# Gated linear attention fused with two expert layers on one core: the states' part of y goes through PSUM columns of its own, ScalarE copies it out and VectorE adds it to the scores' part

## The reference, cut to what matters

```python
f = 1.0 / (1.0 + np.exp(-f_logit))                    # 4 batches, 8 heads, 768 steps, 48 wide
for t in range(S):
    state = f[:, :, t, :, None] * state + np.einsum('bhd,bhe->bhde', k[:, :, t], v[:, :, t])
    y[:, :, t] = np.einsum('bhd,bhde->bhe', q[:, :, t], state)
x = y.transpose(0, 2, 1, 3).reshape(B * S, H * D)     # 3072 tokens, 384 wide
x = (sigmoid(x @ w_gate) * (x @ w_val)) @ w_out       # hidden width 1536
h = x @ w_in                                          # hidden width 2048
out = (h * sigmoid(1.702 * h)) @ w_out2
```

## Time and profile before

| | us |
|---|---|
| median of 3 runs | 974.91 |
| lowest and highest run | 974.26, 975.66 |
| the profiled execution, its time | 974.81 |
| the profiled execution, its span | 973.1 |
| PE busy in that span | 950.0 (98%) |
| DVE, ACT, POOL busy | 491.0, 303.3, 106.0 |
| mean granted PE clock, as a share of 2.4 GHz | 0.991 |

### The profile page before, as it was taken

The page is one execution under the profiler, slowest core; times in us unless marked ns, Lnnn a source line. Parts: engine busy times, 40 slices in busy tenths (PEclk is TensorE's granted clock), DMA queues, the critical chain, the costliest instruction groups (busy, mean ns, idle before and its releaser), DMA issues.

```text
span 973.1 us, 17708 instructions
## 1 busy us (share of the span) xinstructions
PE 950.0 (98%) x7149; PEld 789.3 (81%) x7149; DVE 491.0 (50%) x876; ACT 303.3 (31%) x621; POOL 106.0 (11%) x125
## 2 busy tenths in 40 slices
PE   7899999999999999999999999999999999999997
PEld 4798988888888887888788888888888888888886
DVE  7787876556554755565332234344343443443433
ACT  3353332222222222222223343333333333332222
POOL 3211211111110111011003440000000000000000
PEclk8899999999999999999999999999999999999999
DMA  5651322211211211121022330020010100100000
GB/s 148 187 174 46 97 69 62 62 42 34 82 43 50 76 52 42 42 75 30 10 90 77 106 105 17 1 66 1 1 65 0 35 31 1 65 1 1 32 1 35
DMA packets 44005, 52.33 MB, mean 54 GB/s; under 512 B 8464, under 2 KB 33808, under 8 KB 43920
## 3 DMA queue, kind: packets, MB, share of 16 engines
q1 hardware_dynamic: 41168, 43.29, 15.3%
q10 hardware_dynamic: 2752, 7.87, 2.7%
HBM read 36.96 MB, written 9.44 MB: 48 GB/s over the span
## 4 chain that ended last, share of the span: by engine, by line
PE 90%; DVE 4%; issue 2%; SPq 1%; ACT 1%; DMA 0%; DVEq 0%
PE up_ps L966 16%; PE up_ps L968 16%; PE up_ps L967 16%; PE out_ps L966 12%; PE out_ps L968 11%; PE out_ps L967 11%; PE att_ps L959 3%; PE att_ps L926 2%; PE att_ps L948 1%; PE turn_ps L905 1%; PE att_ps L938 1%; DVE w_lo L766 1%; ACT act_hi L630 1%; DVE prod L712 1%; DVE act_f L814 0%
## 5 line engine op out<-in xcount | busy, mean ns | idle before, releaser
L966 PE MATMUL up_ps<-x_hi,w_hi 128*128 128x512 f32 (+1 forms) x792 | 294.5, 372 | 5.2 <-DVE x_lo L759 2.7
L968 PE MATMUL up_ps<-x_hi,w_lo 128*128 128x512 f32 (+1 forms) x792 | 293.0, 370 | 0.0
L967 PE MATMUL up_ps<-x_lo,w_hi 128*128 128x512 f32 (+1 forms) x792 | 293.0, 370 | 0.0
L966 PE MATMUL out_ps<-act_hi,w_hi 128*128 128x512 f32 (+1 forms) x540 | 208.5, 386 | 0.7 <-DVE act_lo L821 0.7
L968 PE MATMUL out_ps<-act_hi,w_lo 128*128 128x512 f32 (+1 forms) x540 | 203.3, 376 | 0.0
L967 PE MATMUL out_ps<-act_lo,w_hi 128*128 128x512 f32 (+1 forms) x540 | 203.0, 376 | 0.0
L630 ACT CAST act_hi<-act_f 128x512 fp32r<-128x512 f32 (+1 forms) x180 | 106.5, 592 | 260.9 <-DVE act_f L814 188.5
L821 DVE TENSOR_TENSOR act_lo<-act_f,act_hi 128x512 fp32r<-128x512 f32 (+1 forms) x180 | 118.5, 658 | 118.5 <-ACT act_hi L630 118.5
L966 PEld LDWEIGHTS up_ps<-x_hi,w_hi 128*128 128x128 f32 x792 | 149.4, 189 | 33.1 <-DVE act_f L814 3.3
L967 PEld LDWEIGHTS up_ps<-x_lo,w_hi 128*128 128x128 f32 x792 | 149.5, 189 | 25.4
L968 PEld LDWEIGHTS up_ps<-x_hi,w_lo 128*128 128x128 f32 x792 | 149.3, 189 | 25.3
(11 more groups left out here) (68 smaller groups left out, 509.9 us busy)
## 6 DMA issues: line engine op xcount, KB each, us to landing
stage<-w SPq DMA_DIRECT2D x16, 384.0 KB, 3.3
stage<-w ACTq DMA_DIRECT2D x9, 576.0 KB, 4.0
q_raw<-q_t SPq DMA_DIRECT2D x96, 48.0 KB, 1.9
k_raw<-k_t SPq DMA_DIRECT2D x96, 48.0 KB, 1.9
v_raw<-v_n SPq DMA_DIRECT2D x48, 96.0 KB, 2.2
x_raw<-x_dram SPq DMA_DIRECT2D x6, 768.0 KB, 4.8
out_t<-final SPq DMA_DIRECT2D x18, 256.0 KB, 2.3
f_raw<-f_t SPq DMA_DIRECT2D x80, 48.0 KB, 1.9
```

What stands on the lines that cost most here:

```text
L966: pe.matmul(dst, w_hi[:, at:at + P], m_hi, start=first, stop=False)
L967: pe.matmul(dst, w_hi[:, at:at + P], m_lo, start=False, stop=False)
L968: return pe.matmul(dst, w_lo[:, at:at + P], m_hi, start=False, stop=last)
```

## The change

`turn_ps[:, 256:512]`, the half of the transposes' bank that was not used, becomes the place of the states' part. A new function `from_states` issues the 8 matmuls of state and `q_dec` there, each with `start=True`; for the first chunk of a sequence they read a tile of zeros, `no_state`, so they are always 8. The wait on PE's own matmuls is dropped, and `visit_done` is raised ahead of them, behind the scores. In its place `from_states` waits for `k_rows_done` of the unit that this visit turned, since the copy of the transposed k reads the same bank, and for ACT's copy of the states' part of the unit before. The transposes wait for that copy too.

ACT's `take_y` becomes `begin_y`: it copies the 256 columns of `turn_ps` into `y_t` behind `states_used`. DVE gets a new instruction per unit, `make_y`, which adds the scores' part from `att_ps` onto `y_t` in place. It stands last in `after_visit`, behind the mask and the states. The mask no longer waits for y. SP's `move_y` waits for `y_done` in place of `y_taken`.

```diff
+                def from_states(n, v):
+                    u = Unit(n)
+
+                    pe.wait_ge(k_rows_done, len([a for a, _, _ in VISITS[:v + 1] if a is not None]))
+                    pe.wait_ge(state_done, states_before(n + 1))
+                    wait(pe, y_begun, n)
+                    for c in range(CH):
+                        before = state_before(u, c) if u.third or c else no_state[:, :]
+                        for i in range(PAIR):
+                            last = pe.matmul(turn_ps[rows[i], W + c * C:W + (c + 1) * C], before[rows[i], :],
+                                             q_dec[rows[i], n % 4, c * C:(c + 1) * C], start=True, stop=True)
+                    last.then_inc(states_used, 1)
...
                         wait(pe, k_rows_done, turned)
+                        wait(pe, y_begun, len([c for _, _, c in VISITS[:v] if c is not None]))
...
+                    last.then_inc(visit_done, 1)
                     if made is not None:
-
-                        last.then_inc(tiles_done, 1)
-                        pe.wait_ge(tiles_done, made + 1)
-                        pe.wait_ge(state_done, states_before(made + 1))
-                        for c in range(0 if m.third else 1, CH):
-                            at = slice(Y_COL + c // SIDES * C, Y_COL + (c // SIDES + 1) * C)
-                            for i in range(PAIR):
-                                last = pe.matmul(ps[rows[i], c % SIDES, at], state_before(m, c)[rows[i], :],
-                                                 q_dec[rows[i], made % 4, c * C:(c + 1) * C], start=False, stop=False,
-                                                 skip_group_check=True)
-                    last.then_inc(visit_done, 1)
+                        from_states(made, v)
...
-                def take_y(n):
+                def begin_y(n):
                     u = Unit(n)
-                    act.wait_ge(visit_done, out_visit[n] + 1)
+                    act.wait_ge(states_used, n + 1)
                     wait(act, y_moved[n % YS], 16 * moves(n % YS, n))
-                    act.copy(y_t[:, n % YS, :].rearrange("p (c r t) -> p c r t", c=BLOCKS, r=SIDES),
-                             banks(out_visit[n])[:, :, Y_COL:Y_COL + BLOCKS * C].rearrange("p r (c t) -> p c r t", c=BLOCKS)).then_inc(y_taken, 1)
+                    act.copy(y_t[:, n % YS, :], turn_ps[:, W:2 * W]).then_inc(y_begun, 1)
...
+                def make_y(n, v):
+                    dve.wait_ge(y_begun, n + 1)
+                    y = y_t[:, n % YS, :].rearrange("p (c r t) -> p r c t", c=BLOCKS, r=SIDES)
+                    own = banks(v)[:, :, Y_COL:Y_COL + BLOCKS * C].rearrange("p r (c t) -> p r c t", c=BLOCKS)
+                    dve.tensor_tensor(y, y, own, ALU.add).then_inc(y_done, 1)
...
                     dve.wait_ge(visit_done, v + 1)
-                    if made is not None:
-                        dve.wait_ge(y_taken, made + 1)
                     if turned is not None:
                         mask(turned, v)
                     if kept is not None:
                         new_states(kept, v)
+                    if made is not None:
+                        make_y(made, v)
...
-                    sp.wait_ge(y_taken, n + 1)
+                    sp.wait_ge(y_done, n + 1)
```

More of the change, by code:

```diff
@@ L598, in _ @@
                 first_load_f(6)
-                take_y(0)
                 load_w1(1)
+                begin_y(0)
                 take_k(3)
@@ L635, in _ @@
                         if made is not None:
-                            take_y(made)
+                            begin_y(made)
                     if b.first_mlp and (b.g, b.j) in FORGET_AT:
@@ L802, in _ @@
                 after_visit(4)
+                after_visit(5)
+                after_visit(6)
                 prepare(4)
```

29 lines of the change are left out of this document (15 added, 14 removed).

## The result

The changed kernel takes 1011.51 us (median of 5 runs, 1009.71 to 1011.93) where the kernel before takes 974.91 (974.05 to 976.36). The ratio is 1.0366, with a 95% interval of 1.0354 to 1.0378. The profiled execution has a span of 1009.8 us at a mean granted clock of 0.983. The prediction was 1007 us, with a range of 999 to 1020 and a range of its own for the forecast of 1001 to 1011. So the direction and the mechanism held, and the size was 4.2 us short of the 36.6: the time lies inside the range and just above the forecast's own.

A forecast was written before the change was run, and what follows sets the result against it. PE, 98% busy, was taken as the bound. The terms 18.9 + 0.9 - 0.6 + 5.9 + 4.3 + 2.3 + 0.7 = 32.4 us on 974.8 made 1007 us, range 999 to 1020.

The forecast's parts named there:

- The wait in the thirty long visits: Groups 2 to 5: the states' matmuls wait for ACT's copy of k, 0.63 us later each, +18.9 us.
- Two matmuls more, the last two visits: Eight made units beginning a sequence take 0.11 us more each, +0.9 us; two visits turning no unit win 0.30 each, -0.6.
- The mask: DVE's mask in group 1 starts right behind the low part, losing its 0.89 us of waiting for y.
- Group 1: Eight visits of 256-token blocks: PE tied to DVE's pace, f loads later by 1.1 us; +5.9 us, from 3.5 to 8.
- Group 0: Four visits with a y: product to product becomes a 5.39 us loop, 1.08 us more each, +4.3 us, lower end 1.3.
- the clock: Group 0: PE stands still until the copy, then runs 27 matmuls at 1.2 GHz once; +2.3 us, from 0 to 9 more.
- The start: Activations wait for moves of y, which now wait for two adds of 0.35 us on DVE; +0.7 us, from 0 to 1.5.
- The copy isn't the last to come: Rival: the copy of k ends early enough that 42 visits win up to 0.30 us each; 962 us, 3%.
- Groups 0 and 1 absorb their part: Rival: the start and groups 0 and 1 cost nothing, only 19.2 us remain; 994 us, 6%.
- The clock falls in every long visit: Rival: PE's clock falls in all thirty long visits at 2.3 us each, 69 us; 1076 us, 5%.
- The clock falls in several short visits: Rival: two to four more losses of 2.3 us in groups 0 and 1; 1012 to 1017 us, 20%.
- At no cost: The other adds, 0.35 us on DVE, lie under PE's work in the long blocks; SP's loads nearly slip in group 1.

The follow-up runs named there:

- e1: The kernel before with one wait added: the states' matmuls wait for ACT's copy of the turned k; 1015.01 us, 1.0396 of before.
- e3: The changed kernel with ACT's copy of k moved ahead of its wait for DVE's product and the cast of act_hi; 976.4 us, 1.0008 of before.
- e12: The changed kernel with ACT's copy of k moved early in groups 2 to 5 alone; 983.18 us, 1.0077 of before.
- e4: The changed kernel with the states' matmuls moved behind the 9 output matmuls that follow the visit; 985.81 us, 1.0104 of before.
- e6: The changed kernel with the early copy of k and SP's loads of f, v, q and k ahead of the move of y; 984.53 us, ratio 1.0098.
- e7: The changed kernel with SP's loads of f, v, q and k ahead of the move of y; 1029.09 us, ratio 1.0549.
- e10: The changed kernel with the early copy of k and only the loads of f ahead of the move of y; 967.93 us, ratio 0.9928.
- e2: The kernel before with a DVE add of zeros onto y per unit, SP's move of y waiting for it; 982.33 us, 1.0073 of before.
- e9: The kernel before for units 0 to 15, the changed kernel's path with the early copy of k for 16 to 47; 967.4 us, ratio 0.9915.

## Why the prediction was right, point by point

**The wait in the thirty long visits: right.** Forecast 0.63 us each and +19.2 with its two small terms; measured 1.15 - 0.52 = 0.63 us in the visit shown, and +19.45. The start behind the signal was 0.05 us (0.06 taken). That it is the copy was shown twice: added alone it brings the loss (e1), moved away it takes the loss with it (e3, e12).

**Two matmuls more, the last two visits: right.** The last visits were to win 0.30 us each and won 0.27, 0.53 us before (484.61 to 485.14) and 0.26 after from the scores' part to the states:

```profile
521.47 0.44 PE L949 MATMUL att_ps<-scores,v_raw 64*48 64x64 f32 x16
521.73 0.63 PE L916 MATMUL turn_ps<-q_dec,state 48*48 48x64 f32 x16
```

The eight visits of groups 2 to 5 whose made unit begins a sequence took 0.47 us from the states to the next output matmul before and take 0.58 now, like all others: the forecast +0.9.

**The mask: right.** It starts right behind the low part in group 1, where it had waited 0.89 us for y:

```profile
101.78 0.42 DVE L831 TENSOR_TENSOR act_lo<-act_f,act_hi 128x256 fp32r<-128x256 f32 x1 [0.47 <-ACT act_hi L629]
102.12 0.42 DVE L732 TENSOR_TENSOR scores<-att_ps,causal 128x256 f32<-128x256 f32 x1
```

**Group 1: right in its steps, short by a fall of the clock.** The walk from product to product was 47.4 us plus 1.1 for f, and measured 150.75 - 100.89 = 49.9. By parts: block 0 6.78 (6.76 forecast); from block 1 to 3 10.48 (9.00), where the fall at 109.2 lies; 3 to 4 5.77 (5.76); 4 to 5 6.22 (5.76); 5 to 7 9.01 (9.00); 7 to 8 5.47 (5.76); 8 to 9 6.13 (5.39). The 0.46 and 0.74 us too many are the two places where the gate waits 3.16 and 3.07 us for f, 1.2 us against the 1.1 put down. The 1.48 us are the clock.

**Group 0: the term that was mis-sized is the clock, in number and in price.** The loop of 5.39 us without it stood in the sum, with one fall of 2.3 in it. Measured were three visits of 6.75, 6.85 and 6.85 us, so three falls of 1.4 to 1.5 us over 5.39: 4.3 + 3 x 1.43 = 8.6, the measured +8.6, where 6.6 was forecast. The number was put at one because the trace before showed one, though PE was to stand still in all four visits; the prediction said that it could not read this, and e12 shows that it differs between executions. The price was too high for an error in the working: the counts of 11 and 20 are of the matmuls that touch the stretch, not of those that fit in it. So 27 at full speed were put at 2.8 us, while the loop that they were added to holds 5.39 - 1.20 - 0.58 = 3.6 for them. The other figure came out by luck: the 27 matmuls behind the states took 63.05 + 0.58 to 68.72, 5.09 us, close to the 5.2 forecast, but that had all of them slow at 0.19 us, and in the trace 16 were slow, at 0.21 (64.80 to 68.18, 3.38 us, where 16 x 0.12 = 1.92 would do at the higher clock). The fourth visit shows the 3.6: from 86.56 + 0.58 to 90.74 it is 3.60 us, and 5.35 for its loop, the forecast of 5.39. 5.09 - 3.60 is 1.5. Three falls instead of one, and one in group 1, at the right price are 4 x 1.45 - 2.3 = 3.5 of the 4.2 us that the prediction was short.

**The start: +1.1 against +0.7.** The wait of the activations became shorter, 2.16 us against 3.49, but it ends at 34.60 in place of 33.51. The size is loose: in the six other runs with the same code up to there (e3, e4, e6, e7, e10, e12) group 0 starts at 36.8 to 37.5 us.

**The rivals.** "The copy isn't the last to come" would have come to 962 us. e3 makes just that true, and PE's visit wins 0.27 us, close to the 0.30 of that rival; it ended at 976.4 and not at 962 because of f and the clock in the short groups, which the rival left out. With both put right (e10) it is 967.9, and the rest is the start and group 0, where nothing was won, and the zeros. "Groups 0 and 1 absorb their part" fell: they cost 16.0 us. "The clock falls in every long visit" fell: the granted clock of groups 2 to 5 is 1.00 although PE stands still 0.72 us or more in thirty visits. "The clock falls in several short visits" is what happened, three more of them, and at the 1012 us that it named for two; that the time fits so well is in part luck, since each cost 1.4 to 1.5 us and not 2.3.

**"At no cost" held for what it spoke of,** the adds in the long blocks: e2 leaves groups 2 to 5 at 356.0. What it said of SP's slipping loads held only for the changed kernel. There the waits for f are 11.9 us in all; in e2 and e3 they are 35.4 and 38.2. Where the slower PE gives the queue more time, the fault of the queue is smaller. How much of the 16 us in groups 0 and 1 the order of f alone would give back in the changed kernel was not run.

**What stays open.** The change gives the states' part half of a bank that the transposes use, and with that the wait. All eight banks are given out, so a real bank of its own was not tried, nor the shared bank without the wait. The Trainium skill (PSUM — Partial Sum Buffer, section "PSUM bank collisions raise a hardware error") asks for the separation by bank and quadrant; no run here shows it. Nor do the runs show what decides whether the clock falls behind such a wait.

## What to carry to other kernels

When an edit drops a wait, look at what stands in its place and which signal comes last there: 0.30 us were dropped and 0.93 put in, and the culprit was a copy behind an unrelated cast on ACT. Ask next whether the signal can come earlier; moving one copy took back 35 of the 36.6 us, and the loads of f moved in the queue on top of it made it a gain of 7.5 us. In a queue that issues in order, move only such loads ahead as wait for nobody: f alone gave back 4.3 us in group 1, f with v, q and k cost 8 to 18.

## What the runs showed of the hardware that was not expected

- **The clock falls at short waits.** PE stood still for 3.70, 1.90 and 1.89 us ahead of the states of three visits of group 0 and worked at 1.2 GHz a little later, and once in group 1 behind a wait of 1.64 us. But behind a fourth wait of 1.89 us (86.56) it went on at 2.4 GHz, while in e12, with the same code there, it was at 1.2 GHz behind that one too (1.91 us). So the length of this wait alone doesn't decide it. The waits in the thirty long visits, 0.72 us and one of 1.07, were never followed by a fall. The Trainium skill (TensorE: Matmul & The Clock Gate, section "HAM oscillation — how this bites in real kernels") describes falls behind gaps between bursts of matmuls. The runs agree in kind, with falls behind waits of 1.64 to 3.70 us.
- **A fall costs only what isn't covered.** Before, group 0 had one fall and took 53.84 us; e9, with the same code there and no fall, took 53.87. DVE set the pace, so it cost nothing. With PE setting the pace a fall cost 1.4 to 1.5 us.
- **Going between small and full matmuls takes time.** A full 128x512 matmul follows another at 0.24 us, but at 0.34 where it is the second behind a set of 48-row ones (e4, e3), and a set of them starts 0.32 us behind a full one (e4).
- **A wait on PE's own matmuls goes with 0.27 us** between two sets of small ones (from scores to states 0.52 us with it before, 0.25 without it in e3), though the engine has nothing else to wait for. The states' tile changed along with the wait, and no run parts the two.
